# A third set of head tiles, with the low halves and the exponential's scale and bias moved to VectorE

## The chip, the cores and the metric

The kernel runs on one core of one Trainium2 chip. The metric is the device time of one execution in microseconds (us). The kernel before takes 824.26 us, the median of three runs (823.79 to 824.98).

## What is computed

Attention with a bucket mask over 2 x 8 heads of 768 positions and 64 dimensions, then two layers on its result (1536 tokens x 512):

```python
q_bits = (q @ proj > 0); k_bits = (k @ proj > 0)          # 6 bits each, a bucket number per position
scores = where(q_bucket == k_bucket, q @ k.T / 8, -1e9)
attn   = softmax(scores); x = attn @ v
h = x @ w_in;  g = (a0 + a1 h + a2 h^2 + a3 h^3) / (1 + |b0||h| + |b1| h^2);  x = g @ w_out
h = x @ w_in2; g = h * clip(h + 3, 0, 6) / 6;                                 out = g @ w_out2
```

Everything is fp32. The products of scores and of the layers are taken as sums of products of halves: a number is split into a rounded upper half (`hi`, type fp32r) and the rest (`lo`).

## The kernel before, in words

Five engines run programs of their own: TensorE (PE), VectorE (DVE), ScalarE (ACT), GpSimd (POOL) and SyncE (SP), which issues every DMA. Each program is written out in its order, and counting semaphores tie them together. There is no planner.

**Heads and tiles.** A head has six tiles of 128 query rows (`TILES`). Two heads are a pair, so there are eight pairs (0 to 7) and 96 tiles (n). Within a pair the tiles are j = 0 to 11, and j = 6 is the first tile of the second head; t is the tile within its head. The loop of every engine is `for i in pairs: for j in 12: step(i, j)`.

**One tile.** PE makes the scores of 128 x 768 into one of two score buffers `s_ps` (lines 775 to 779), once the exponential of tile n-2 has freed it. DVE takes the negated maximum (L595). POOL makes from it the scale (L378) and the bias (L381) of the exponential. ACT takes the exponential with its row sum (L432). DVE inverts the sum (L601), POOL multiplies by it (L387). Three tiles later (`TURN_LAG`) PE transposes the result (L786), and ACT and DVE each copy one half of it out of PSUM (L443, L611). In pair i PE also multiplies the transposed probabilities of pair i-1 by v (`weigh`, L803), in three pieces per head at t = 1, 3 and 5.

**Preparing a head.** The scores need four operand tiles per head: `q_main`, `k_main` (upper halves, with twelve more rows of signed mask bits) and `q_cross`, `k_cross` (which pair upper with lower halves). Before, there are two sets of them, one for each head of a pair. `raw` holds q in its partitions 0 to 63 and k in 64 to 127. ACT makes the upper half (`split_hi`, L426) at t = 0 of the head before, POOL the lower half (`split_lo`, L369) at t = 1. A DMA has to carry the parts to other partitions: SP's `place_head` (L261) issues three moves, waits until they have landed, and issues a fourth; `place_bits` (L275) issues four moves of mask bits. The bits come from `project` on PE (L763, at j = 7 for the next pair) and `threshold` on DVE (L590, at j = 8). The first scores of a head wait for all five DMAs of `main_in`.

**SP's order.** SP waits in order, so what stands behind a wait is late with it. Its loop over the heads h is: `place_head(h+1)`, v of the pair, an early load of weights, `place_bits(h+1)`, the next `raw`.

**Early weights.** The upper and lower halves of the first layer's weights are made in slots; before, five slots (`EARLY_SLOTS`) are made during pairs 2 to 6, one per pair: SP loads `w_raw` at the head of the pair, ACT takes the upper half at j = 4 and j = 8 (L459, `EARLY_AT`), and waits there until the load has landed. POOL makes the lower half (L394). The other slots are made in the first layer's first chunk.

**Layers.** After pair 7, PE runs 96 steps, each with `hidden` (L823 to L825) and `outputs` (L876).

Of the kernel before, what the change touches and what calls it, by code (L numbers as in the profile page):

```python
# [27 lines left out]
P = 128  # L28
# [5 lines left out]
def bucket_attention_and_two_mlps(nc, q, k, v, proj, w_in0, w_out0, poly_a, poly_b, w_in1, w_out1, out):  # L34
# [55 lines left out]
    with ctx:  # L90
# [29 lines left out]
        FREE_SLOTS = 5  # L120
# [5 lines left out]
        with attn:  # L126
            raw = [[sb(f"raw{e}{u}", [P, SEQ], F32, attn) for u in range(2)] for e in range(2)]
            pt_first = [[None, None], [None, None]]
            for g in range(2):
# [3 lines left out]
                for u in range(2)])  # L133
# [28 lines left out]
        bit_col_in = sem("bit_col_in")  # L162
        sel_made = sem("sel_made")
# [5 lines left out]
        v_in = [sem(f"v_in{e}") for e in range(2)]  # L169
        hi_made = sem("hi_made")  # L170
# [3 lines left out]
        moved_in = [sem(f"moved_in{u}") for u in range(2)]  # L174
        main_in = [sem(f"main_in{u}") for u in range(2)]
# [51 lines left out]

        def early_half(i, j):
# [16 lines left out]
        def _(sp):  # L245
# [14 lines left out]

            def place_head(h):  # L261

                u = h % 2
                sp.wait_ge(hi_made, h + 1)
                move(k_main[u][0:D, :], q_main[u][D:P, :]).then_inc(moved_in[u], 16)
                move(k_cross[u][0:D, :], q_main[u][D:P, :]).then_inc(moved_in[u], 16)
                if h > 0:
                    sp.wait_ge(lo_made, h + 1)
                    move(k_cross[u][D:P, :], q_cross[u][D:P, :]).then_inc(moved_in[u], 16)
                    sp.wait_ge(moved_in[u], 48 * (h // 2 + 1) - (16 if u == 0 else 0))  # L270
                move(q_cross[u][D:P, :], q_main[u][0:D, :]).then_inc(main_in[u], 16)
                if h == 0:
                    sp.wait_ge(moved_in[u], 32)

            def place_bits(h):  # L275

                i, u = divmod(h, 2)
                sp.wait_ge(bits_made, i + 2 if h else 1)
                for half in range(2):
                    cols = slice(HALF * half, HALF * (half + 1))  # L280
                    at = QUAD * (2 * u + half)
                    move(q_main[u][D:KROWS, cols], bits[at:at + MASKROWS, :]).then_inc(main_in[u], 16)
                    move(k_main[u][D:KROWS, cols], bits[at + MASKROWS:at + 2 * MASKROWS, :]).then_inc(main_in[u], 16)
# [11 lines left out]
            load_raw(0, 0)  # L295
            sp.dma_start(proj_raw[0:D, :], proj).then_inc(proj_in, 16)
            sp.dma_start(proj_raw[D:P, :], proj).then_inc(proj_in, 16)
            load_raw(0, 1)
            sp.wait_ge(sel_made, 4)
            for c in range(2):  # L300
                sp.dma_start(bit_col[:, c:c + 1], bit_row[0:1, c, :]).then_inc(bit_col_in, 16)
            place_head(0)
            load_v(0)
            place_bits(0)
            load_raw(1, 0)
            load_raw(1, 1)
            sp.dma_start(a_col[:, :], poly_a.partition_broadcast(P)).then_inc(poly_in, 16)
            sp.dma_start(b_raw[:, :], poly_b.partition_broadcast(P)).then_inc(poly_in, 16)

            for h in range(NHEAD):  # L310
                i, u = divmod(h, 2)
                if h + 1 < NHEAD:
                    place_head(h + 1)
                if u == 0 and i >= 1:
# [5 lines left out]
                if h >= 1 and h + 3 < NHEAD:  # L320
                    sp.wait_ge(lo_made, h)
                    sp.wait_ge(bits_dot, (h - 1) // 2 + 2)
                    load_raw((h + 3) // 2, (h + 3) % 2)
# [20 lines left out]
        def _(pool):  # L344
# [20 lines left out]
            def split_lo(h):  # L365

                u = h % 2
                alone(hi_made, h + 1)
                nc.gpsimd.tensor_tensor(q_cross[u][:, :], raw[h // 2 % 2][u][:, :], q_main[u][:, :].bitcast(F32),  # L369
                                        ALU.subtract).then_inc(lo_made, 1)  # L370

            def bias(n, j):


                r = j % 4
                neg = neg_max[:, r:r + 1]
                alone(maxed, n + 1)
                nc.gpsimd.tensor_scalar(exp_scale[:, r:r + 1], neg, MATCHED, SCALE, ALU.is_lt, ALU.mult)\  # L378
                    .then_inc(matched, 1)
                alone(matched, n + 1)  # L380
                nc.gpsimd.tensor_scalar(exp_bias[:, r:r + 1], neg, exp_scale[:, r:r + 1], 1.0, ALU.mult, ALU.mult)\  # L381
                    .then_inc(biased, 1)

# [13 lines left out]
            pool.wait_ge(lo_made, 1)  # L397
            for i in range(PAIRS):
                for j in range(2 * TILES):
                    h, n = 2 * i + j // TILES, 2 * TILES * i + j  # L400
                    bias(n, j)
                    if n >= 1:
                        normalise(n - 1, j - 1)
                    if j % TILES == 1 and h + 1 < NHEAD:
                        split_lo(h + 1)
# [11 lines left out]
        def _(act):  # L417

            nc.scalar.preload_act_table_set("natural_log_exp_and_others")
# [41 lines left out]
            def step(i, j):  # L461
# [8 lines left out]
                if t == 0 and h + 1 < NHEAD:  # L470
                    split_hi(h + 1)
# [459 lines left out]
```

## Time and profile before

| | us |
|---|---|
| Median of 3 runs | 824.26 (823.79 to 824.98) |
| The profiled execution | 824.72 |
| Its span, first to last instruction | 822.5 |
| PE busy | 769.8 (94%) |
| DVE busy | 465.1 (57%) |
| ACT busy | 439.0 (53%) |
| POOL busy | 240.4 (29%) |
| First scores | 15.28 |
| First `hidden` | 280.64 |

The busy time of PE counts matmuls with modelled ends and is no measure of its idle time; for that one reads where a matmul starts and what released it. The first 281 us are attention, where the engines work by turns; the rest is dense on PE.

### The profile page before, as it was taken

To read this page: it belongs to the slowest core of one execution; us is meant where nothing else is said; L and a number is where in the kernel's file an instruction comes from. 1 tells how busy PE (TensorE), PEld (TensorE's weight loads), DVE (VectorE), ACT (ScalarE), POOL (GpSimd) and SP (SyncE) were. 2 spreads that over 40 slices of the span, in tenths; PEclk is the share of its full clock that TensorE was granted. 3 is DMA by queue.
4 is the path that set the end of the run, shared out by engine and by line. 5 is a ranking of instruction groups with operands and counts; after the bars stand their busy time and mean duration, and the time that the engine had idled before them with its cause. 6 is when DMAs were issued, how large, how long until landed. Compare 5 with 4: busy or idle time off the path is not lost.

```text
span 822.5 us, 11290 instructions
## 1 busy us (share of the span) xinstructions
PE 769.8 (94%) x3712; PEld 595.7 (72%) x3712; DVE 465.1 (57%) x777; ACT 439.0 (53%) x781; POOL 240.4 (29%) x379
## 2 busy tenths in 40 slices
PE   3889898798979799999999999999999999999998
PEld 1665565465655558888888888888888888888886
DVE  3656565465645458888988898984222322232223
ACT  1656665576656648877766688984221222212221
POOL 1756676576756414420000024443000000000000
PEclk9989999989989999999999999999999999999999
DMA  5233434434333002320000013331000100000001
GB/s 147 53 91 84 126 75 116 112 87 115 93 98 88 1 26 84 96 77 0 1 0 0 0 31 99 101 103 52 1 0 1 51 0 0 0 34 18 1 1 51
DMA packets 35451, 43.50 MB, mean 53 GB/s; under 512 B 4496, under 2 KB 23696, under 8 KB 35408
## 3 DMA queue, kind: packets, MB, share of 16 engines
q1 hardware_dynamic: 35408, 42.95, 19.1%
q8 instruction: 24, 0.39, 0.2%
q14 instruction: 19, 0.16, 0.1%
HBM read 26.22 MB, written 3.15 MB: 36 GB/s over the span
## 4 chain that ended last, share of the span: by engine, by line
PE 78%; DMA 7%; SPq 5%; POOL 4%; DVE 3%; issue 2%; ACT 1%; POOLq 0%; ACTq 0%; DVEq 0%
PE y_ps L876 32%; PE h_ps L823 11%; PE h_ps L824 11%; PE h_ps L825 11%; PE o_ps L803 4%; PE t_ps L786 4%; DMA k_cross<-q_cross 3%; PE s_ps L776 3%; SPq L259 3%; PE s_ps L777 2%; DMA k_main<-bits 2%; POOL q_cross L369 2%; DVE neg_max L595 2%; POOL probs L387 1%; SPq L255 1%
## 5 line engine op out<-in xcount | busy, mean ns | idle before, releaser
L823 PE MATMUL h_ps<-x_hi,slot 128*128 (+1 forms) x384 | 149.7, 390 | 1.5 <-DVE x_lo L617 1.5
L824 PE MATMUL h_ps<-x_lo,slot 128*128 (+1 forms) x384 | 149.4, 389 | 0.0
L825 PE MATMUL h_ps<-x_hi,slot 128*128 (+1 forms) x384 | 149.4, 389 | 0.0
L394 POOL TENSOR_TENSOR slot<-w_raw,slot 128x512 fp32r<-128x512 f32 x64 | 81.7, 1294 | 215.6 <-ACT slot L459 215.5
L672 DVE SCALAR_TENSOR_TENSOR t_abs<-t_abs,h_ps 128x512 f32<-128x512 f32 x48 | 33.0, 688 | 187.2 <-ACT t_abs L496 187.2
L496 ACT ACTIVATE t_abs<-h_ps,three_col 128x512 f32<-128x512 f32 x48 | 33.1, 690 | 192.1 <-PE h_ps L825 192.1
L595 DVE TENSOR_REDUCE neg_max<-s_ps 128x1 f32<-128x768 f32 x96 | 91.7, 955 | 76.7 <-PE s_ps L777 76.5
L432 ACT ACTIVATE probs<-s_ps,exp_bias,exp_scale 128x768 f32<-128x768 f32 x96 | 95.2, 991 | 62.0 <-POOL exp_bias L381 61.1
L876 PE MATMUL y_ps<-g_hi,slot 128*128 128x512 f32 x384 | 126.1, 389 | 0.0
L876 PE MATMUL y_ps<-slot,g_hi 128*128 128x512 f32 x384 | 118.2, 389 | 0.0
L776 PE MATMUL s_ps<-k_cross,q_cross 128*128 128x512 f32 x192 | 80.0, 417 | 36.2 <-DMA k_main<-bits 24.3
L786 PE MATMUL t_ps<-ident,probs 128*128 128x128 f32 x576 | 90.9, 291 | 6.0 <-ACT pt_second L443 3.2
L387 POOL TENSOR_SCALAR probs<-probs,row_inv 128x768 f32<-128x768 f32 x96 | 87.5, 911 | 20.1 <-DVE row_inv L601 19.7
L776 PEld LDWEIGHTS s_ps<-k_cross,q_cross 128*128 128x128 f32 x192 | 39.9, 208 | 72.7 <-DMA k_main<-bits 33.3
L823 PEld LDWEIGHTS h_ps<-x_hi,slot 128*128 128x128 f32 x384 | 72.1, 188 | 17.3 <-DVE x_lo L617 1.8
L876 PEld LDWEIGHTS y_ps<-g_hi,slot 128*128 128x128 f32 x384 | 72.1, 188 | 15.4 <-DVE g_lo L678 0.2
L825 PEld LDWEIGHTS h_ps<-x_hi,slot 128*128 128x128 f32 x384 | 72.0, 188 | 15.1
L876 PEld LDWEIGHTS y_ps<-slot,g_hi 128*128 128x128 f32 x384 | 72.0, 188 | 14.9
L824 PEld LDWEIGHTS h_ps<-x_lo,slot 128*128 128x128 f32 x384 | 72.1, 188 | 14.7
L786 PEld LDWEIGHTS t_ps<-ident,probs 128*128 128x128 f32 x576 | 70.9, 150 | 13.3 <-issue 12.5
L876 PE MATMUL y_ps<-g_lo,slot 128*128 128x512 f32 x192 | 74.7, 389 | 0.0
L876 PE MATMUL y_ps<-slot,g_lo 128*128 128x512 f32 x192 | 74.7, 389 | 0.0
(68 smaller groups left out, 1189.0 us busy)
## 6 DMA issues: line engine op xcount, KB each, us to landing
w_raw<-in_moe_w_in SPq DMA_DIRECT2D x32, 256.0 KB, 2.7
w_raw<-in_moe_w_out SPq DMA_DIRECT2D x32, 256.0 KB, 2.8
raw<-in_q SPq DMA_DIRECT2D x16, 192.0 KB, 3.1
raw<-in_k SPq DMA_DIRECT2D x16, 192.0 KB, 3.3
k_main<-q_main SPq DMA_DIRECT2D x16, 192.0 KB, 2.5
k_cross<-q_main SPq DMA_DIRECT2D x16, 192.0 KB, 2.9
q_cross<-q_main SPq DMA_DIRECT2D x16, 192.0 KB
v_nat<-in_v SPq DMA_DIRECT2D x16, 192.0 KB, 2.7
```

Of the source, the lines that this page charges most:

```text
L387: nc.gpsimd.tensor_scalar(probs[j % 4][:, :], probs[j % 4][:, :], row_inv[:, r:r + 1], 1.0, ALU.mult, ALU.mult).then_inc(normed, 1)
L394: nc.gpsimd.tensor_tensor(slots[f][:, j, 1, :], w_raw[j][:, :], slots[f][:, j, 0, :].bitcast(F32), ALU.subtract).then_inc(w_lo_made, 1)
L432: nc.scalar.activation(probs[j % 4][:, :], s_ps[j % 2][:, 0:SEQ], ACT.Exp, scale=exp_scale[:, r:r + 1], bias=exp_bias[:, r:r + 1], accum_o ...
L496: nc.scalar.activation(t_abs[b][:, :], h_ps[b][:, :], ACT.Relu, bias=three_col[:, :])\
L595: nc.vector.tensor_reduce(neg_max[:, j % 4:j % 4 + 1], s_ps[j % 2][:, 0:SEQ], AX.X, ALU.max, negate=True)\
L672: nc.vector.scalar_tensor_tensor(t_abs[b][:, :], t_abs[b][:, :], 6.0, h_ps[b][:, :], ALU.min, ALU.mult).then_inc(g_made, 1)
L776: mm(s_ps[j % 2][:, c0:c1], q_cross[u][:, rows], k_cross[u][:, c0:c1], start=True, stop=False)
L786: last = nc.tensor.transpose(t_ps[half][:, P * s:P * (s + 1)], probs[n % 4][:, c:c + P], ident[:, :])
L823: mm(h_ps[b][:, :], w_hi, x_hi[:, kt, cols], start=(kt == 0), stop=False)
L824: mm(h_ps[b][:, :], w_hi, x_lo[:, kt, cols], start=False, stop=False)
L825: last = mm(h_ps[b][:, :], w_lo, x_hi[:, kt, cols], start=False, stop=(kt == KT - 1))
L876: last = mm(y_ps[d][:, :], still, moving, start=(f == 0 and a == 0), stop=(f == FT - 1 and a == 2))
```

## The change

- There are three sets of head tiles (`SETS = 3`), taken in turn by the head's number. Every step of the preparation moves one head earlier: during head h, head h+2 is made ready. `project` moves from j = 7 to j = 1 and `threshold` from j = 8 to j = 2.
- `split_lo` and `bias` (the scale and bias) move from POOL to DVE. The bias stands right behind the maximum.
- SP's loop over h becomes: v, the whole of `place_head(h+2)` with its bits (two moves of k bits ahead of the wait for the landing, two moves of q bits behind it), `raw` of h+6, and then the early weights.
- One slot of weights less fits: `EARLY_SLOTS` 4, made in pairs 3 to 6.
- The first head is made without moves between partitions: q and k are also loaded swapped into `raw[1][0]`, and ACT and DVE copy from there. ACT issues some of the first DMAs. `raw` of heads 2 and 3 is loaded behind `place_head(1)`.
- At the end the transposes of tile 93 go ahead of the first `hidden`, and the copies of turned tiles go earlier on ACT and DVE; the last x but two is made at j = 10 in place of 11.

```diff
-    PROJECT_AT = TILES + 1
+    PROJECT_AT = 1
+    SETS = 3
-    LAST_X = {5: 2 * PAIRS - 4, 11: 2 * PAIRS - 3}
-    EARLY_SLOTS = 5
+    LAST_X = {5: 2 * PAIRS - 4, 10: 2 * PAIRS - 3}
+    EARLY_SLOTS = 4
...
+            def place_keys(h):
+                c = h % SETS
                 sp.wait_ge(hi_made, h + 1)
+                move(k_main[c][0:D, :], q_main[c][D:P, :]).then_inc(moved_in[c], 16)
+                move(k_cross[c][0:D, :], q_main[c][D:P, :]).then_inc(moved_in[c], 16)
+            def place_head(h):
+                c = h % SETS
+                place_keys(h)
+                sp.wait_ge(bits_made, h // 2 + 2)
+                place_bits(sp, h, 1)
+                sp.wait_ge(lo_made, h + 1)
+                move(k_cross[c][D:P, :], q_cross[c][D:P, :]).then_inc(moved_in[c], 16)
+                sp.wait_ge(moved_in[c], moved(h))
+                move(q_cross[c][D:P, :], q_main[c][0:D, :]).then_inc(main_in[c], 16)
+                place_bits(sp, h, 0)
...
+            place_bits(sp, 0, 0)
             load_v(0)
-            place_bits(0)
+            place_head(1)
+            sp.wait_ge(first_k, 2)
             load_raw(1, 0)
             load_raw(1, 1)
+            load_raw(2, 0)
+            load_raw(2, 1)
...
             for h in range(NHEAD):
                 i, u = divmod(h, 2)
-                if h + 1 < NHEAD:
-                    place_head(h + 1)
                 if u == 0 and i >= 1:
                     load_v(i)
+                if h + 2 < NHEAD:
+                    place_head(h + 2)
+                if h + 6 < NHEAD:
+                    load_raw((h + 6) // 2, h % 2)
                 if u == 0 and EARLY_PAIR <= i < EARLY_PAIR + EARLY_SLOTS:
                     load_weights(0, i - EARLY_PAIR)
-                if h + 1 < NHEAD:
-                    place_bits(h + 1)
...
 (ACT)
-                if t == 0 and h + 1 < NHEAD:
-                    split_hi(h + 1)
+                if t == 0 and h + 2 < NHEAD:
+                    split_hi(h + 2)
...
+            act.wait_ge(swapped_in, 32)
+            for to in (k_main, k_cross):
+                nc.scalar.activation(to[0][0:D, :], raw[1][0][0:D, :], ACT.Copy).then_inc(first_k, 1)
...
             act.wait_ge(hi_made, 1)
+            split_hi(1)
...
 (DVE)
                 maximum(n, j)
+                bias(n, j)
                 if n >= 1:
                     invert(n - 1, j - 1)
...
                 if j == PROJECT_AT + 1 and i + 1 < PAIRS:
                     threshold(i + 1)
+                if t == 1 and h + 2 < NHEAD:
+                    split_lo(h + 2)
...
 (PE, behind the last step)
+            for half in range(2):
+                turn_probs(NTILE - 3, half)
             hidden(0, 0, 0, 0)
-            for n in (NTILE - 3, NTILE - 2):
-                for half in range(2):
-                    turn_probs(n, half)
+            for half in range(2):
+                turn_probs(NTILE - 2, half)
```

**SP, pair 3 (its v load to the `raw` load of the second head's turn).** Before:

```order
67 L255 DMA v_nat<-in_v 128x384 [waits pv_done]
68 L255 DMA v_nat<-in_v 128x384
69 L293 DMA w_raw<-in_moe_w_in 128x4x128
70 L293 DMA w_raw<-in_moe_w_out 128x512
71 L259 DMA q_main<-bits 12x384 [waits bits_made]
72 L259 DMA k_main<-bits 12x384
```

With the change, the same place (v of pair 3, then head 8's moves):

```order
83 L267 DMA v_nat<-in_v 128x384 [waits pv_done]
84 L267 DMA v_nat<-in_v 128x384
85 L271 DMA k_main<-q_main 64x768 [waits hi_made]
86 L271 DMA k_cross<-q_main 64x768
87 L287 DMA k_main<-bits 12x384 [waits bits_made]
88 L287 DMA k_main<-bits 12x384
89 L271 DMA k_cross<-q_cross 64x768 [waits lo_made]
90 L271 DMA q_cross<-q_main 64x768 [waits moved_in2]
91 L287 DMA q_main<-bits 12x384 x2
92 L260 DMA raw<-in_q 64x768
93 L261 DMA raw<-in_k 64x768
94 L309 DMA w_raw<-in_moe_w_in 128x4x128
```

The weights stood right behind v; now they stand behind nine or ten more issues and behind four waits, of which `bits_made` is the threshold at j = 2 of the same pair.

**ACT, the first rows with the change, up to the first exponential (L429).**

```order
7 L477 ACTIVATE k_main<-raw 64x768 [waits swapped_in]
8 L477 ACTIVATE k_cross<-raw 64x768
9 L481 DMA k_main<-bits 12x384 [waits bits_made]
10 L481 DMA k_main<-bits 12x384
11 L423 ACTIVATE q_main<-raw 128x768 [waits raw_in01,hi_made]
12 L423 ACTIVATE q_main<-raw 128x768 [waits raw_in10]
13 L429 ACTIVATE probs,row_sum<-s_ps,exp_bias,exp_scale 128x768 [waits biased] x3
```

Before, the first exponential stood right behind row 11's counterpart; now a second split, of head 2, which waits for `raw[1][0]`, stands ahead of it.

**DVE, one tile with the change (t = 1 of the second head, with `split_lo` behind it).**

```order
44 L599 TENSOR_REDUCE neg_max<-s_ps 128x1 [waits scored]
45 L608 TENSOR_SCALAR exp_scale<-neg_max 128x1 [waits maxed]
46 L611 TENSOR_SCALAR exp_bias<-neg_max,exp_scale 128x1 [waits matched]
47 L616 RECIPROCAL row_inv<-row_sum 128x1 [waits exped]
48 L626 COPY pt_first<-t_ps 128x3x128 [waits turned]
49 L594 TENSOR_TENSOR q_cross<-raw,q_main 128x768 [waits hi_made]
```

Before, a tile on DVE was the first, fourth and fifth of these rows; the second, third and (once per head) the last are new there.

## Rows read from the trace of the kernel before

**Rows 1.** What PE waited for, 0 to 330 us: total us, times, longest.

```profile
PE s_ps L776 <- DMA k_main<-bits: 24.3, 8, 6.7
```

**Rows 2.** PE's timeline: start us, us, line, tile [idle before <-releaser].

```profile
46.09 0.80 PE L776 MATMUL s_ps<-k_cross,q_cross 128*128 128x512 f32 x1 [3.52 <-DMA k_main<-bits]
...
53.46 0.50 PE L776 MATMUL s_ps<-k_cross,q_cross 128*128 128x512 f32 x1
...
96.29 0.47 PE L776 MATMUL s_ps<-k_cross,q_cross 128*128 128x512 f32 x1 [3.37 <-DMA k_main<-bits]
...
102.23 0.85 PE L763 MATMUL p_ps<-raw,proj_pair 128*32 128x384 f32 x8
103.01 0.50 PE L776 MATMUL s_ps<-k_cross,q_cross 128*128 128x512 f32 x1
...
112.09 0.50 PE L776 MATMUL s_ps<-k_cross,q_cross 128*128 128x512 f32 x1
...
117.14 0.50 PE L776 MATMUL s_ps<-k_cross,q_cross 128*128 128x512 f32 x1
...
129.27 0.47 PE L776 MATMUL s_ps<-k_cross,q_cross 128*128 128x512 f32 x1 [2.98 <-ACT probs L432]
...
136.27 0.50 PE L776 MATMUL s_ps<-k_cross,q_cross 128*128 128x512 f32 x1
...
247.86 0.50 PE L776 MATMUL s_ps<-k_cross,q_cross 128*128 128x512 f32 x1
```

**Rows 3.** The window view: us, then busy us of PE to POOL, granted clock, DMA.

```profile
46.00:52.00 6.00, 5.91 (x22) 5.01 (x24) 2.99 (x6) 2.06 (x4) 1.68 (x5) 0.50 0.45 123
```

**Rows 4.** Timeline of SP and ACT in pair 3 (SPq: an issue).

```profile
123.61 0.44 SPq L293 DMA_DIRECT2D w_raw<-in_moe_w_in  x1
...
124.65 0.81 SPq L259 DMA_DIRECT2D q_main<-bits  x1
...
127.53 0.63 ACT L459 ACTIVATE slot<-w_raw 128x512 fp32r<-128x512 f32 x1 [4.00 <-DMA w_raw<-in_moe_w_in]
...
128.46 0.60 SPq L249 DMA_DIRECT2D raw<-in_k  x1
```

**Rows 5.** DMA issues, 118 to 152 us: KB each, median us from issue to landing.

```profile
k_cross<-q_cross SPq DMA_DIRECT2D x2, 192.0 KB, 2.5
...
raw<-in_k SPq DMA_DIRECT2D x2, 192.0 KB, 3.3
...
w_raw<-in_moe_w_in SPq DMA_DIRECT2D x1, 256.0 KB, 3.9
```

**Rows 6.** The page's DMA issues: the same load over the whole span.

```profile
w_raw<-in_moe_w_in SPq DMA_DIRECT2D x32, 256.0 KB, 2.7
```

**Rows 7.** DVE's timeline: two rows of one tile, and the threshold behind project.

```profile
79.75 0.96 DVE L595 TENSOR_REDUCE neg_max<-s_ps 128x1 f32<-128x768 f32 x1 [0.91 <-PE s_ps L777]
80.62 0.15 DVE L601 RECIPROCAL row_inv<-row_sum 128x1 f32<-128x1 f32 x1
...
81.15 0.55 DVE L611 COPY pt_second<-t_ps 128x384 f32<-128x384 f32 x1
...
105.43 0.67 DVE L590 TENSOR_SCALAR bits<-p_ps,bit_col 128x384 fp32r<-128x384 f32 x1
```

**Rows 8.** The timeline of the first 24 us.

```profile
16.94 0.96 DVE L595 TENSOR_REDUCE neg_max<-s_ps 128x1 f32<-128x768 f32 x1 [7.44 <-PE s_ps L777]
...
18.83 0.99 ACT L432 ACTIVATE probs<-s_ps,exp_bias,exp_scale 128x768 f32<-128x768 f32 x1 [10.81 <-POOL exp_bias L381]
```

**Rows 9.** The end of attention: PE's timeline, and of the chain that ended last its L803.

```profile
263.84 0.50 PE L776 MATMUL s_ps<-k_cross,q_cross 128*128 128x512 f32 x1 [1.75 <-DMA k_main<-bits]
...
278.14 0.97 PE L786 MATMUL t_ps<-ident,probs 128*128 128x128 f32 x6
...
294.35 0.88 PE L786 MATMUL t_ps<-ident,probs 128*128 128x128 f32 x6
...
297.99 4.02 PE p_ps L803 x24
```

More of the change, by code:

```diff
@@ L132, in bucket_attention_and_two_mlps @@
                 [sb(f"{name}{u}", [P, SEQ], F32R, attn) for name in ("q_cross", "k_cross", "q_main", "k_main")]
-                for u in range(2)])
+                for u in range(SETS)])
             bits = sb("bits", [P, HALF], F32R, attn)
@@ L173, in bucket_attention_and_two_mlps @@
         bits_made = sem("bits_made")
-        moved_in = [sem(f"moved_in{u}") for u in range(2)]
-        main_in = [sem(f"main_in{u}") for u in range(2)]
+        first_k = sem("first_k")
+        moved_in = [sem(f"moved_in{s}") for s in range(SETS)]
+        main_in = [sem(f"main_in{s}") for s in range(SETS)]
         scored = sem("scored")
@@ L259, in move, with place_bits @@
                 return sp.dma_start(dst.bitcast(F32), src.bitcast(F32))
[L261 to L263 removed]
+            def place_keys(h):
+                c = h % SETS
                 sp.wait_ge(hi_made, h + 1)
[L265 to L278, printed above, removed]
+                move(k_main[c][0:D, :], q_main[c][D:P, :]).then_inc(moved_in[c], 16)
+                move(k_cross[c][0:D, :], q_main[c][D:P, :]).then_inc(moved_in[c], 16)
+            def place_bits(queue, h, side):
+                c, at = h % SETS, 2 * QUAD * (h % 2) + MASKROWS * side
+                to = (q_main, k_main)[side][c]
                 for half in range(2):
                     cols = slice(HALF * half, HALF * (half + 1))
[L281 to L283 removed]
+                    rows = slice(at + QUAD * half, at + QUAD * half + MASKROWS)
+                    queue.dma_start(to[D:KROWS, cols].bitcast(F32), bits[rows, :].bitcast(F32)).then_inc(main_in[c], 16)
+            def place_head(h):
[8 more added lines that the diff above has]
+                place_bits(sp, h, 0)
             def load_weights(m, f):
@@ L363, in _ @@
                                     base=0, pattern=[[-1, P]], channel_multiplier=1).then_inc(sel_made, 1)
[L365 to L382, printed above, removed]
             def normalise(n, j):
@@ L417, in _ @@
         def _(act):
+            act.dma_start(raw[0][0][D:P, :], k_dram[dram_head(0, 0), :, :]).then_inc(raw_in[0][0], 16)
+            act.dma_start(proj_raw[0:D, :], proj).then_inc(proj_in, 16)
+            act.dma_start(raw[1][0][0:D, :], k_dram[dram_head(0, 0), :, :]).then_inc(swapped_in, 16)
+            act.wait_ge(sel_made, 4)
+            for c in range(2):
+                act.dma_start(bit_col[:, c:c + 1], bit_row[0:1, c, :]).then_inc(bit_col_in, 16)
             nc.scalar.preload_act_table_set("natural_log_exp_and_others")
@@ L424, in split_hi @@
                 act.wait_ge(raw_in[i % 2][u], 32 * (i // 2 + 1))
-                after(act, scored, TILES * (h - 1))
-                nc.scalar.activation(q_main[u][:, :], raw[i % 2][u][:, :], ACT.Copy).then_inc(hi_made, 1)
+                after(act, scored, TILES * (h - SETS + 1))
+                nc.scalar.activation(q_main[h % SETS][:, :], raw[i % 2][u][:, :], ACT.Copy).then_inc(hi_made, 1)
             def exponentials(n, j):
@@ L476, in step @@
                     split_weights(0, f, (half,))
+            act.wait_ge(swapped_in, 32)
+            for to in (k_main, k_cross):
+                nc.scalar.activation(to[0][0:D, :], raw[1][0][0:D, :], ACT.Copy).then_inc(first_k, 1)
+            act.wait_ge(bits_made, 1)
+            for half in range(2):
+                cols, rows = slice(HALF * half, HALF * (half + 1)), QUAD * half + MASKROWS
+                act.dma_start(k_main[0][D:KROWS, cols].bitcast(F32), bits[rows:rows + MASKROWS, :].bitcast(F32))                    .then_inc(main_in[0], 16)
             act.wait_ge(hi_made, 1)
+            split_hi(1)
             for i in range(PAIRS):
@@ L775, in scores @@
                 for c0, c1 in ((0, BANK), (BANK, SEQ)):
-                    mm(s_ps[j % 2][:, c0:c1], q_cross[u][:, rows], k_cross[u][:, c0:c1], start=True, stop=False)
-                    last = mm(s_ps[j % 2][:, c0:c1], q_main[u][0:KROWS, rows], k_main[u][0:KROWS, c0:c1],
+                    mm(s_ps[j % 2][:, c0:c1], q_cross[c][:, rows], k_cross[c][:, c0:c1], start=True, stop=False)
+                    last = mm(s_ps[j % 2][:, c0:c1], q_main[c][0:KROWS, rows], k_main[c][0:KROWS, c0:c1],
                               start=False, stop=True)
@@ L849, in _ @@
             pe.wait_ge(x_ready, 2 * PAIRS - 2)
+            for half in range(2):
+                turn_probs(NTILE - 3, half)
             hidden(0, 0, 0, 0)
-            for n in (NTILE - 3, NTILE - 2):
-                for half in range(2):
-                    turn_probs(n, half)
+            for half in range(2):
+                turn_probs(NTILE - 2, half)
             weigh(PAIRS - 1, 0, tuple(range(TILES)))
```

75 lines of the change are left out of this document (47 added, 28 removed).

## The prediction

> **What bounds the kernel now.** I read the waits of PE first, then PE's timeline at the heads' first tiles, then the engines behind each wait. Behind attention PE runs without a gap and the change leaves its work alone, so every gain or loss lies in attention. There PE's largest wait is for `k_main<-bits`, the last DMA of a head's placing: 24.3 us in 8 waits [rows 1]. The pattern is: the second head of pair 2 starts at 96.29 after 3.37 us of idleness, while from 103.01 to 112.09 four tiles take 9.08, or 4.54 per two tiles, with no wait at all [rows 2]. So without waits PE's own work is the bound: 6 x 4.54, plus 0.78 for project (102.23 to 103.01), plus 0.5 at a pair's first two tiles (112.09 to 117.14 is 5.05), **28.5 us for a pair**. Pairs 1 and 2 together take 66.0 (46.09 to 112.09), pairs 3 to 6 together 135.8 (112.09 to 247.86) [rows 2].
>
> A second wait hides behind the first. In pair 3 the second head starts at 129.27, released not by a DMA but by ACT's exponential [rows 2]. ACT had stood 4.00 us at j = 4 for the early weights, which SP issued at 123.61, 11.5 us behind the pair's first scores; they landed at 127.53, and 1.74 us later (half a split, then the exponential of tile 4) PE went on [rows 2, 4]. Such a wait costs more than its length: the two tiles from 129.27 to 136.27 take 7.00, less 0.78 for project 6.2, against 4.54. After the wait at 46.09 the granted clock stood at 0.50, the lower level of 1.2 GHz, from the first tile [rows 3], and two tiles took 7.4 (to 53.46).
>
> **The change part by part.** Times below are from PE's first scores of the pair, S.
>
> *Third set of tiles.* Per pair SP has about 20 us of issues and landings (two heads at 8.7, v, weights), under 28.5, and begins a head early, so a head's placing is ready with over 10 us to spare. The waits for bits go. Pairs 1 and 2, which have no early weights now, become 2 x 28.5 = 57.0: **-9.0**.
>
> *Early weights.* They now stand behind all of `place_head(h+2)` and `raw`. The gate is the threshold at j = 2. Project begins at S+5.05 on PE's pace; from project to the end of the threshold are 3.20 + 0.67 (102.23 to 105.43) [rows 2, 7], and 0.34 for two small operations now ahead of it: S+9.3. Then SP issues two k bits (0.81 each, with gaps 1.66) [rows 4], and a move that lands 2.5 after its issue [rows 5]: S+13.4. Then 0.5 for the last move, 1.66 for two q bits, and 1.2 for `raw` in pairs 3 and 4 (0.60 each) [rows 4]; `raw` of h+6 ends with head 15, so pairs 5 and 6 have none. The weights are issued at S+16.8 and S+15.6, against 11.5 now. They land 3.9 later in pair 3's row [rows 5], 2.7 in the median over the span, mostly without other traffic [rows 6]; I take 3.9 behind `raw` and 3.3 without: S+20.7 and S+18.9. With the 1.74 of ACT, tile 6 starts at S+22.4 and S+20.6, some 7 and 5 us after PE has run out of work. For the restart the bounds are 6.2 and 7.4 [rows 2]. I take 7.4, because that row's clock was already down when PE resumed, as it should be after a longer wait. The last four tiles take 9.1, as from 103.01 to 112.09. So pairs 3 and 4 take 38.9 and pairs 5 and 6 37.1, together 152.0 against 135.8: **+16.2**. What is saved at heads is more than given back here.
>
> *Bias and low halves on DVE.* Today the exponential starts 1.89 behind the maximum's start (16.94 to 18.83) [rows 8]. On DVE two small operations of 0.15, each behind a wait on its own engine of some 0.03, make it about 1.4. In steady pairs this is worth nothing, because PE's own work ends last. DVE's load per tile, start to start, is 0.87 for the maximum, 0.07 for the reciprocal and 0.46 for the copy of 0.55 [rows 7], 1.4 in all, and becomes 1.8; a head adds 0.95 for the low half, a pass over 768 columns as the maximum is [rows 8], and 0.8 for the rest, or 12.6 against PE's 14.2. It is hidden, with 1.6 to spare. If that cover goes, each us too much per head costs up to 14 us.
>
> The Trainium skill, "VectorE: DVE Perf Modes", section "The DRAIN you can't avoid", says that the next operation does not start until the pipe is empty, and that a semaphore between two adds nothing. By full spans a tile costs 2.0 and a head 13.6, still under PE's, and pair 0, where DVE ends last, would be 2 us longer: the sum would be 821. The trace speaks against the first half: the reciprocal starts at 80.62, while the maximum lasts to 80.71 [rows 7].
>
> *Start.* q, k and the bits go in without moves, and the first scores could start near 10.4. But ACT must split head 2 before the first exponential, and that waits for `raw[1][0]`. SP issues it only behind `place_head(1)`. On the same durations: threshold at 7.4; two bits to 9.1, v to 10.0, two moves to 11.2, two bits to 12.8, a landing at 15.3, a move and two bits to 17.5, k issued at 18.1, landed 3.3 later [rows 5] at 21.4. The split takes 0.85, so the first exponential starts at 22.25, not 18.83 [rows 8]: 3.4 later. From it to pair 1's first scores are 27.3 today, 4.3 of them waits for bits (0.82 at the second head, 3.52 at 46.09) [rows 2]. The shorter way to the exponential gives 0.5 on each of six rounds of two tiles, DVE's two low halves take 1.7 back. 22.25 + 27.3 - 4.3 - 1.3 = 43.9, against 46.09: **-2.2**. Bounds: 42 and 46.
>
> *Pair 7 and the end.* Its second head waits 1.75 [rows 9] and restarts at the lower clock (1.7 by 6.2 less 4.54): **-3.4**. Today the transposes end at 278.8, and then PE waits for x, and twice for turned tiles behind ACT's and DVE's reading of `hidden`, until tile 95 is transposed at 294.35. With the new order the same work is: 0.4 for the normalised tile 93, 3.64 for six transposes and a `hidden` (294.35 to 297.99), 0.7 for six more, 4.02 for 24 matmuls of `weigh` [rows 9], or 287.5: **-6.9**. Below nothing it can't come; half of it is the other bound. One slot less is ready at the first layer; the others follow one per step of 5.44 us and lie some 6 us ahead of their use, so it costs nothing. If the first were later by more than that, PE would wait for each.
>
> Sum: -2.2 - 9.0 + 16.2 - 3.4 - 6.9 = -5.3. The profiled execution took 824.72 (span 822.5), 0.5 above the median; 824.26 - 5.3 gives **819.0**.
>
> **Rivals.**
> - *Still later weights: slower.* At ACT's wait at j = 4 of pairs 3 to 6. Each us by which the weights land later costs 4 us; from 1.3 us on, S+22, the kernel is slower than before. A threshold held up by DVE's larger load (up to 1) and 1 us more to land than in the row make 2 us: 827. For it speaks that four waits stand ahead; against it, that DVE has slack then.
> - *The wait for weights is hidden.* If PE had other work, pairs 3 to 6 would take 28.5 each, and the time would be 819 - 38 = 781. Against it stands 129.27, released by the exponential right behind the split [rows 2].
> - *DVE starts nothing before the operation ahead has ended.* Then a tile costs 2.0 there, and pair 0 is 2 us longer: 821. Against it: 80.62 lies before 80.71 [rows 7].
> - *No difference.* Half of the end's gain and the start's fail to come (+4.5): 823.5.
> - *The change doesn't do what it says.* Heads still wait for bits, since SP is one queue. Against it: 20 us of work in 28.5. Such waits would lie inside the weights' wait in pairs 3 to 6, so only pairs 1 and 2 lose their 9.0: 828.
>
> **How the numbers follow.** A difference within 0.2% (822.6 to 825.9) can't be told from none. The forecast has 0.60: its own range is 810 (restarts at 6.2, -4.8, and weights 1 us earlier, -4) to 824 (start and end at their other bounds). DVE held back has 0.05, at 821; that is the skill's DRAIN rule. Later weights have 0.17, no difference 0.11, heads that still wait 0.03, the hidden wait 0.04. The range, 808 to 828, leaves out the hidden wait and the far ends. Of the forecast 0.03 lies in "same". Faster 0.57 + 0.05 + 0.04 = 0.66, same 0.14, slower 0.20.
>
> **What would show it.** In the new profile: no wait for bits from tile 6 on; four waits of ACT for `w_raw` of 7 to 9 us, and behind each a wait of PE for the exponential of 5 to 8 us; weights issued 15 to 17 us behind the pair's first scores; the first scores near 10.4 but the first exponential at 22; pairs 1 and 2 at 28.5 each, DVE near 12.6 busy us per head. The prediction is wrong if the four waits are short, if pairs 1 and 2 take over 30 us (then DVE bounds), or if the first layer waits for slots.

## The result and the profile after

The changed kernel takes **834.8 us**, the median of four runs (833.84 to 835.36), against 824.62 for the kernel before, measured beside it (four runs, 823.79 to 828.26). The ratio is 1.0118, with a 95% interval of 1.0100 to 1.0135: slower by 1.2%, or 10.2 us between the medians. The prediction, 819.0 in a range of 808 to 828, had the wrong sign. The profiled execution took 835.36 us.

The page of the changed kernel: the span, the busy times, and in 40 slices the granted clock of PE.

```profile
span 833.6 us, 11076 instructions
...
PE 769.8 (92%) x3712; PEld 591.5 (71%) x3712; DVE 514.5 (62%) x985; ACT 439.1 (53%) x783; POOL 170.6 (20%) x172
...
PEclk9999998979899999999999999999999999999999
```

PE is busy for the same 769.8 us as before, in a span that is 11.1 us longer; POOL has lost 70 us of work and DVE has gained 49. So what counts is where PE stood. PE's timeline of the changed kernel, in the columns of [rows 2]: the first scores of pairs 1, 2 and 3, the second head of pair 3, its third tile, pair 4, pair 7, the first `hidden` and the first `outputs`.

```profile
47.90 0.47 PE L810 MATMUL s_ps<-k_cross,q_cross 128*128 128x512 f32 x1
...
79.28 0.51 PE L810 MATMUL s_ps<-k_cross,q_cross 128*128 128x512 f32 x1
...
110.98 0.50 PE L810 MATMUL s_ps<-k_cross,q_cross 128*128 128x512 f32 x1
...
133.58 0.77 PE L810 MATMUL s_ps<-k_cross,q_cross 128*128 128x512 f32 x1 [6.38 <-ACT probs L429]
...
140.02 0.51 PE L810 MATMUL s_ps<-k_cross,q_cross 128*128 128x512 f32 x1
...
150.02 0.50 PE L810 MATMUL s_ps<-k_cross,q_cross 128*128 128x512 f32 x1
...
265.34 0.50 PE L810 MATMUL s_ps<-k_cross,q_cross 128*128 128x512 f32 x1
...
297.83 0.48 PE L857 MATMUL h_ps<-x_hi,slot 128*128 128x512 f32 x1
...
315.91 0.39 PE L911 MATMUL y_ps<-g_hi,slot 128*128 128x512 f32 x1
```

In the trace of the kernel before, the first `outputs` row is this one:

```profile
304.83 0.39 PE L876 MATMUL y_ps<-g_hi,slot 128*128 128x512 f32 x1
```

Read with [rows 2], these rows divide the 11.1 us between the two traces among four stretches, and leave nothing for the fifth:

| stretch | before | after | difference | predicted |
|---|---|---|---|---|
| start, to pair 1's first scores | 46.09 | 47.90 | +1.8 | -2.2 |
| pairs 1 and 2 | 66.00 | 63.08 | -2.9 | -9.0 |
| pairs 3 to 6 | 135.77 | 154.36 | +18.6 | +16.2 |
| pair 7, to the first `outputs` | 56.97 | 50.57 | -6.4 | -10.3 |
| from there to the end | 517.7 | 517.7 | 0.0 | 0.0 |

Two waits stand behind this table. PE's and ACT's waits of the changed kernel from 0 to 330 us, in the columns of [rows 1]:

```profile
ACT slot L456 <- DMA w_raw<-in_moe_w_in: 27.8, 4, 8.2
PE s_ps L810 <- ACT probs L429: 23.1, 5, 6.7
...
PE t_ps L820 <- DVE pt_first L626: 8.4, 18, 1.5
PE t_ps L820 <- DVE pt_second L626: 7.8, 20, 0.8
...
PE s_ps L810 <- DMA k_main<-bits: 4.1, 1, 4.1
```

The waits for bits are down from 8 to 1, the very first. In their place stand four waits of ACT for `w_raw`, of about 7 us each, with PE behind it at the exponential: that was forecast. The 38 waits of PE's transposes for DVE's copies, 16.2 us in all, were not.

The first of the two in pair 3. SP's issues and ACT's half of the weights, from the timeline of the changed kernel:

```profile
120.74 1.59 SPq L287 DMA_DIRECT2D k_main<-bits  x2
...
128.33 0.59 SPq L309 DMA_DIRECT2D w_raw<-in_moe_w_in  x1
...
131.84 0.63 ACT L456 ACTIVATE slot<-w_raw 128x512 fp32r<-128x512 f32 x1 [7.84 <-DMA w_raw<-in_moe_w_in]
```

From the pair's first scores (110.98) the k bits go out at 9.8, the weights at 17.4, ACT gets them at 20.9, and tile 6 starts at 22.6. The prediction had 9.3, 16.8, 20.7 and 22.4.

The second, in a steady pair. DVE, ACT and PE in one tile of pair 2 of the changed kernel, in order of time:

```profile
86.52 0.96 DVE L599 TENSOR_REDUCE neg_max<-s_ps 128x1 f32<-128x768 f32 x1 [1.14 <-PE s_ps L811]
...
87.51 0.15 DVE L608 TENSOR_SCALAR exp_scale<-neg_max 128x1 f32<-128x1 f32 x1
...
87.69 0.49 PE L820 MATMUL t_ps<-ident,probs 128*128 128x128 f32 x3
87.70 0.21 DVE L611 TENSOR_SCALAR exp_bias<-neg_max,exp_scale 128x1 f32<-128x1 f32 x1
87.83 0.15 DVE L616 RECIPROCAL row_inv<-row_sum 128x1 f32<-128x1 f32 x1
87.90 0.54 DVE L626 COPY pt_second<-t_ps 128x384 f32<-128x384 f32 x1
87.94 1.00 ACT L429 ACTIVATE probs<-s_ps,exp_bias,exp_scale 128x768 f32<-128x768 f32 x1 [0.61 <-DVE exp_bias L611]
...
88.58 0.52 PE L820 MATMUL t_ps<-ident,probs 128*128 128x128 f32 x3 [0.40 <-DVE pt_second L626]
```

DVE is idle for 1.14 us ahead of the maximum, and yet PE waits for DVE. The copy that frees the transposes' buffer stands behind the maximum and three small operations, so it starts 1.38 us behind the maximum's start, and PE's next three transposes wait 0.40 us for it. DVE has time enough; it is its order that PE meets.

### The profile page after: what moved, and what is told of

Its sections match the earlier page's. It is cut to its first block, busy times and chain, and to the rows that moved or that the text cites. A ratio compares the mean times of both kernels' runs of the same rounds, so it can differ in the third digit from the quotient of the medians.

```text
span 833.6 us, 11076 instructions
## 1 busy us (share of the span) xinstructions
PE 769.8 (92%) x3712; PEld 591.5 (71%) x3712; DVE 514.5 (62%) x985; ACT 439.1 (53%) x783; POOL 170.6 (20%) x172
## 4 chain that ended last, share of the span: by engine, by line
PE 79%; DVE 11%; DMA 4%; SPq 3%; issue 2%; ACT 1%; ACTq 0%; DVEq 0%
PE y_ps L911 31%; PE h_ps L857 10%; PE h_ps L858 10%; PE h_ps L859 10%; PE o_ps L837 6%; DVE neg_max L599 5%; PE t_ps L820 3%; PE s_ps L810 3%; PE s_ps L811 2%; SPq L287 2%; DMA k_cross<-q_cross 2%; DMA w_raw<-in_moe_w_in 1%; DVE pt_first L626 1%; DVE pt_second L626 1%; DVE exp_scale L608 1%
## 5 line engine op out<-in xcount | busy, mean ns | idle before, releaser
L599 DVE TENSOR_REDUCE neg_max<-s_ps 128x1 f32<-128x768 f32 x96 | 91.4, 952 | 42.8 <-PE s_ps L811 42.8
L429 ACT ACTIVATE probs<-s_ps,exp_bias,exp_scale 128x768 f32<-128x768 f32 x96 | 95.2, 991 | 39.5 <-DVE exp_bias L611 38.8
L810 PE MATMUL s_ps<-k_cross,q_cross 128*128 128x512 f32 x192 | 78.8, 410 | 27.5 <-ACT probs L429 23.1
L820 PEld LDWEIGHTS t_ps<-ident,probs 128*128 128x128 f32 x576 | 68.7, 147 | 30.0 <-issue 29.9
```

The source lines that it names most:

```text
L429: nc.scalar.activation(probs[j % 4][:, :], s_ps[j % 2][:, 0:SEQ], ACT.Exp, scale=exp_scale[:, r:r + 1], bias=exp_bias[:, r:r + 1], accum_o ...
L599: nc.vector.tensor_reduce(neg_max[:, j % 4:j % 4 + 1], s_ps[j % 2][:, 0:SEQ], AX.X, ALU.max, negate=True)\
L810: mm(s_ps[j % 2][:, c0:c1], q_cross[c][:, rows], k_cross[c][:, c0:c1], start=True, stop=False)
L820: last = nc.tensor.transpose(t_ps[half][:, P * s:P * (s + 1)], probs[n % 4][:, c:c + P], ident[:, :])
```

## The experiments

The theory after this reading: the four waits for weights come from SP's order alone, and the copy waits from DVE's order alone, not from DVE's load. The rivals: weights would be late in any order; the low halves fill DVE; the bias on DVE is too much work wherever it stands. All experiments are edits of the changed kernel, four to ten runs each, beside runs of the kernel before, whose medians in these batches lay between 824.2 and 825.4.

**Weights first (SP).**

```diff
                 if u == 0 and i >= 1:
                     load_v(i)
+                if u == 0 and EARLY_PAIR <= i < EARLY_PAIR + EARLY_SLOTS:
+                    load_weights(0, i - EARLY_PAIR)
                 if h + 2 < NHEAD:
                     place_head(h + 2)
                 if h + 6 < NHEAD:
                     load_raw((h + 6) // 2, h % 2)
-                if u == 0 and EARLY_PAIR <= i < EARLY_PAIR + EARLY_SLOTS:
-                    load_weights(0, i - EARLY_PAIR)
```

> The changed kernel with one edit: SP loads the early weights right behind v, ahead of place_head(h+2). Theory A (the weights' wait is what pairs 3 to 6 lose, 37.6 to 40.1 us each where pairs 1 and 2 take 31.4 and 31.7): ACT's waits for w_raw vanish, pairs 3 to 6 take 31.7 each, time 834.8 - 27.6 = 807. Rival (the second half of those pairs would wait for something else, the bits of the next heads, which are now issued 1 us later, or for the same exponential): 820 or more, with another wait of PE at tile 6.

Measured: 807.82 us, 0.9798 of before (0.9781 to 0.9815). PE's waits with weights first, 0 to 330 us:

```profile
PE t_ps L820 <- DVE pt_first L626: 9.8, 22, 1.5
PE t_ps L820 <- DVE pt_second L626: 8.3, 21, 0.8
...
PE s_ps L810 <- ACT probs L429: 0.4, 1, 0.4
```

PE's wait for the exponential is gone, 23.1 to 0.4, and the head's placing is not late for it: there is no new wait for bits. Pairs 3 to 6 take 126.8 us in this trace (112.33 to 239.10) instead of 154.4. Two lines moved are worth 27.0 us between the medians. The copy waits are all still there.

**The same from ACT's side.** SP's order stays, and ACT takes the weights at j = 8 and 10.

```diff
-    EARLY_AT = (4, 8)
+    EARLY_AT = (8, 10)
```

> The changed kernel with EARLY_AT (8, 10) in place of (4, 8): SP loads the weights where it did, ACT takes them four and two tiles later. They land at S+20.9, tile 8's turn comes near S+21. If only the lateness against ACT's turn costs, the waits nearly vanish as with the weights first (807.8): 808 to 812. If the load itself disturbs (traffic beside the head's moves), it stays above 815.

Measured: 807.81 us, 0.9807 (0.9769 to 0.9844), the same as with weights first to 0.01 us in the median. ACT's waits for `w_raw<-in_moe_w_in` are gone from its list. So the late load itself cost nothing. What cost was that ACT stood in line for it, with the exponentials behind it. Where one of the two is mended, there is nothing left for the other.

**Copy first (DVE).** The scale and bias stay on DVE, but behind the copy, and so does the reciprocal.

```diff
                 maximum(n, j)
+                if n >= TURN_LAG:
+                    take_turned(n - TURN_LAG)
                 bias(n, j)
...
-                if n >= TURN_LAG:
-                    take_turned(n - TURN_LAG)
```

> The changed kernel with one edit: on DVE the copy of the turned tile stands right behind the maximum, ahead of scale and bias. Theory A (the order on DVE: PE waits 0.4 us for the copy at every second tile, because two small operations stand ahead of it): two tiles take 4.54 again in place of 4.97, PE's waits for pt_first and pt_second of DVE go, pairs 1, 2 and 7 gain 2.6 each and the second halves of pairs 3 to 6 0.9 each, about 12 in all: 823. Rival (DVE has too much work, whatever its order): no change, 834 to 835.

Measured: 820.38 us, 0.9953 (0.9938 to 0.9968), 14.4 under the changed kernel. DVE's timeline with the copy first, one tile of pair 2:

```profile
88.64 0.96 DVE L599 TENSOR_REDUCE neg_max<-s_ps 128x1 f32<-128x768 f32 x1 [0.39 <-PE s_ps L811]
89.51 0.55 DVE L626 COPY pt_first<-t_ps 128x384 f32<-128x384 f32 x1
```

The copy starts 0.87 behind the maximum, not 1.38. Pairs 1 and 2 take 29.0 us each in this trace (48.30, 77.32, 106.36), against 31.5 with the bias first and 28.5 in the prediction, and no wait of PE's transposes for DVE is left in the list. DVE still does all the work that the change gave it. One thing beside the order differs: the low half takes 0.94 us on DVE here and mostly 1.54 in the changed kernel (see the last section). The run with the low halves on POOL, below, shows that this is not what mends the pairs.

**Bias back on POOL.** `bias` moves from DVE's loop into POOL's, ahead of `normalise`; on POOL it is `tensor_scalar` with a second multiplier of 1.0. The calls, without the functions that move with them:

```diff
 (POOL)
+                    bias(n, j)
...
 (DVE)
                 maximum(n, j)
-                bias(n, j)
```

> The changed kernel with scale and bias back on POOL, and nothing else. If their place on DVE costs the 0.4 us at every second tile, PE's waits for DVE's copy go and the time is 823 to 825 (the exponential starts 0.5 later, which is hidden). If the bias on DVE is worth something that I don't see, it is over 835.

Measured: 822.65 us, 0.9971 (0.9960 to 0.9983). Pairs 1 and 2 take 28.9 and 29.0 us. It mends the pairs as copy first does.

**Low halves back on POOL, the bias still on DVE.**

```diff
 (POOL)
+                    if j % TILES == 1 and 2 * i + j // TILES + 2 < NHEAD:
+                        split_lo(2 * i + j // TILES + 2)
...
 (DVE)
-                if t == 1 and h + 2 < NHEAD:
-                    split_lo(h + 2)
```

> The changed kernel with the low halves (split_lo of heads 2 to 15) back on POOL, bias left on DVE. Theory A (order of bias and copy): nearly nothing, 833 to 835, since only one tile per head has the low half behind it. Rival (DVE's load): 14 low halves of 0.9 us off DVE give up to 12 us: 823.

Measured: 833.64 us, 1.0103 (1.0080 to 1.0125), hardly under the changed kernel's 834.8. Pairs 1 and 2 take 31.3 and 31.5 us: taking the low halves from DVE (12 of them, 17.9 us, from 48 to 285 us in the changed kernel) mends next to nothing while the bias stands ahead of the copy. Less load on DVE in its old order leaves the pairs at 31.4, and the same operations in a new order bring them to 29.0: that rules out DVE's load as the cause.

**Both back on POOL.** What is left is the third set with SP's new order, the new start and the new end.

> The changed kernel with both moved pieces back on POOL: scale and bias, and the low halves of heads 2 to 15. What is left of the change is the third set with its order on SP, the start and the end. If the loss of 3 us per pair came from the bias's place alone, this equals the run with only the bias back (822.65): 821 to 824. If the low half on DVE is worth something of its own, it is slower than that by a few us.

Measured: 822.14 us, 0.9982 (0.9960 to 1.0004), no different from the kernel before as far as this tells. Pairs 1 and 2 take 28.8 and 29.0. So without its DVE part the change gives to the heads and the end what it takes elsewhere: in this trace pairs 1 and 2 are 8.1 us shorter than in the kernel before and pair 7 with the end 8.7, while pairs 3 to 6 are 10.0 longer and the start 3.0.

**The old end**: the order of transposes and copies as before, and `LAST_X` back at 11. ACT's and DVE's copies go back to their places too, which is left out here.

```diff
-    LAST_X = {5: 2 * PAIRS - 4, 10: 2 * PAIRS - 3}
+    LAST_X = {5: 2 * PAIRS - 4, 11: 2 * PAIRS - 3}
...
 (PE)
-            for half in range(2):
-                turn_probs(NTILE - 3, half)
             hidden(0, 0, 0, 0)
-            for half in range(2):
-                turn_probs(NTILE - 2, half)
+            for n in (NTILE - 3, NTILE - 2):
+                for half in range(2):
+                    turn_probs(n, half)
```

> The changed kernel with the old order at the end (transposes and copies of tile 93 behind the first hidden, the last x but two at j = 11). From the traces the new order gave 6.1 us between the first hidden and the first outputs (24.35 against 18.24) and about as much as nothing before it: 841. If the order is worth nothing and the difference came from something else: 835.

Measured: 841.89 us, 1.0220 (1.0180 to 1.0261). The end's new order is worth 7.1 us, against the 6.9 of the prediction. (The expectation's 24.35 and 18.24 are 24.19 and 18.08 in the traces, with the same difference.) PE's waits with the old end, from 294 to 325 us:

```profile
PE t_ps L820 <- DVE pt_second L626: 2.1, 2, 1.7
PE t_ps L820 <- ACT pt_second L440: 1.8, 1, 1.8
PE h_ps L857 <- DVE x_lo L632: 1.2, 1, 1.2
```

Of these 5.1 us all but 0.4 are the waits that the prediction named: for x (1.2), and twice for turned tiles behind the reading of `hidden` (1.7 and 1.8). In the changed kernel there are 1.8 us of waits behind 283 us.

**The start: `raw` of heads 2 and 3 ahead of `place_head(1)`.** The second split of ACT stands ahead of the first exponential and waits for it.

```diff
             load_v(0)
-            place_head(1)
             sp.wait_ge(first_k, 2)
+            sp.wait_ge(hi_made, 1)
             load_raw(1, 0)
             load_raw(1, 1)
+            place_head(1)
```

> The changed kernel with the loads of raw[1][0] and raw[1][1] issued ahead of place_head(1). Theory (ACT's split of head 2, ahead of the first exponential, waits for that load): the first exponential starts near 18 in place of 25.06, and all behind it comes 7 us earlier: 828. Rival (place_head(1), now 2.5 us later, makes head 1 late by more): PE waits for bits at tile 6 and half of it is lost, 831.

Measured: 831.21 us, 1.0083 (1.0057 to 1.0110), 3.6 under the changed kernel. First the rows of the changed kernel at its start: the first bits, SP's k of `raw[1][0]`, the second split and the first exponential.

```profile
9.27 1.67 SPq L287 DMA_DIRECT2D q_main<-bits  x2
...
20.84 0.60 SPq L261 DMA_DIRECT2D raw<-in_k  x1
...
24.31 0.84 ACT L423 ACTIVATE q_main<-raw 128x768 fp32r<-128x768 f32 x1 [11.72 <-DMA raw<-in_k]
...
25.06 0.98 ACT L429 ACTIVATE probs<-s_ps,exp_bias,exp_scale 128x768 f32<-128x768 f32 x1
```

And the timeline with `raw` first (its line numbers are one higher, by the added wait):

```profile
17.23 0.97 ACT L430 ACTIVATE probs<-s_ps,exp_bias,exp_scale 128x768 f32<-128x768 f32 x1
...
21.68 1.59 SPq L287 DMA_DIRECT2D q_main<-bits  x2
...
24.62 0.68 DVE L588 TENSOR_SCALAR bits<-p_ps,bit_col 128x384 fp32r<-128x384 f32 x1 [2.22 <-DMA q_main<-bits]
...
27.27 0.87 PE L821 MATMUL t_ps<-ident,probs 128*128 128x128 f32 x3 [2.47 <-DVE pt_first L627]
```

The first exponential comes 7.8 us earlier, at 17.23, but pair 1 only 3.6 earlier, at 44.31. The rest turned into another wait: `place_head(1)` is later by its place on SP, its q bits land late, DVE's threshold waits 2.22 us until the tile of bits is free, and the copy behind it on DVE makes PE wait 2.47. The expectation's 828 was too low for want of that chain; how much of the difference each of its links takes was not tried. The 831 is the number of the expectation's rival, but the wait that the rival named is not there: PE has no wait for bits behind the first.

**Together.** Weights first and copy first:

> The changed kernel with two edits: the weights right behind v on SP, and the copy ahead of the bias on DVE. If the two causes are independent and each pair then runs at PE's own pace (29.0 us as pairs 1 and 2 in the run with the copy first), pairs 1 to 7 and 0 gain what they did apart, and pairs 3 to 6 2.7 each once more over the weights alone: 807.8 - 2.7 * 7 - 1 = 788.

Measured: 789.57 us, 0.9571 (0.9552 to 0.9589). Alone the two gave 27.0 and 14.4 us, together 45.2. The traces show where most of the 3.8 more come from. With weights first the pairs from 1 to 6 take 31.7 us (the first of them 31.9), and with both 29.0, so the copy's order is worth 2.7 in each; with late weights it gave 7.6 in pairs 3 to 6 together (154.4 to 146.8), 1.9 in each, or 3.0 less. The likely reason is that part of a pair's copy waits lay inside PE's wait for the exponential; no run tried that alone. PE's waits with both edits, from 30 to 330 us:

```profile
PE s_ps L810 <- ACT probs L429: 2.9, 6, 0.8
PE t_ps L820 <- ACT pt_second L440: 2.5, 7, 1.1
PE t_ps L820 <- ACT pt_first L440: 1.6, 7, 0.2
```

**Is the bias on DVE worth anything then?** Weights first, with scale and bias on POOL:

> The changed kernel with the weights first on SP (as in e1) and scale and bias back on POOL (as in e3). It tells what making the bias on VectorE is worth once the queue's order is right, against e6 (789.57), where the bias stays on VectorE behind the copy. Theory (the bias only has to be out of the copy's way, and VectorE has a little more room without it): e2 and e3 stood at 820.4 and 822.65, POOL's bias 2.3 behind, so e7 about 792, in 789.5 to 795. Rival (a bias on POOL comes late enough to hold up the exponentials, and once the weights no longer cover it, that shows on every tile): over 797. Other rival (the bias on VectorE buys nothing, and its four small operations there cost): under 788.5.

Measured: 792.69 us, 0.9619 (0.9586 to 0.9652): 3.1 behind the bias on DVE behind the copy. In the traces 2.7 of it are there at the first `hidden` (252.50 against 255.17), and 2.1 by pair 2 (77.75 against 79.83); from there pairs 2 to 6 take 29.0 in both, and pair 7 gives the last 0.7. The shorter way to the exponential pays in pairs 0, 1 and 7, and nothing in a steady pair. In pairs 0 and 1 PE waits for the exponential for 2.9 us with the bias on DVE and 4.8 with it on POOL; what makes the difference in pair 7 was not looked into.

**With `raw` first too:**

> The same two edits and the loads of raw[1] ahead of place_head(1). Expected: the kernel with the two edits less what the loads gave alone, about 7: 781.

Measured: 784.71 us, 0.9512 (0.9492 to 0.9532). The best of the study, 40.3 us under the kernel before as measured beside it (825.02) and 50.1 under the change. Pair 1 starts at 43.27 (48.74 without), and six pairs take 29.0 each. The gain over the two edits is 4.9, where 7 had been expected.

**And the projection's matrix loaded first,** on both queues, since PE's first project had waited for it. SP's part; ACT's is alike:

```diff
+            sp.dma_start(proj_raw[D:P, :], proj).then_inc(proj_in, 16)
             sp.dma_start(raw[0][0][0:D, :], q_dram[dram_head(0, 0), :, :]).then_inc(raw_in[0][0], 16)
             sp.dma_start(raw[1][0][D:P, :], q_dram[dram_head(0, 0), :, :]).then_inc(swapped_in, 16)
-            sp.dma_start(proj_raw[D:P, :], proj).then_inc(proj_in, 16)
```

> The same three edits, and proj ahead of raw on both queues at the start. In the changed kernel proj landed at 6.39, 1.4 later than before, behind five loads of 192 KB; first in its queues it should land near 3.5, project then waits for raw alone (about 5), and everything comes 1.5 to 2 us earlier than with the three edits. If raw then lands later by as much, nothing is gained.

Measured: 785.50 us, 0.9522 (0.9503 to 0.9541): a miss, no gain. Of its timeline, DVE's copy of the matrix and the first move of bits:

```profile
2.96 0.51 DVE L580 TENSOR_SCALAR proj_pair<-proj_raw 64x6 f32<-64x6 f32 x4 [2.06 <-DMA proj_raw<-in_proj]
...
9.83 1.68 SPq L287 DMA_DIRECT2D q_main<-bits  x2
```

The matrix is there 3.2 us earlier (2.96, and 6.15 without the edit), and now q and k are late: PE's project waits for them until 5.51 and again for 1.9 us. The q bits go out at 9.83, and at 9.03 without the edit.

## Why the prediction was wrong

**Third set of tiles: right.** No wait for bits is left but the first, and a head's placing stays out of the way even with the weights ahead of it on SP. The rival that heads still wait for bits falls.

**Early weights: right in mechanism, +18.6 for +16.2.** Weights issued, landed and tile 6 started within 0.6 us of the working, and the second heads of pairs 3 to 6 start at 22.6, 23.0, 20.6 and 20.7 us (22.4 and 20.6 predicted). The restart at the lower clock took 6.4 in pair 3 (133.58 to 140.02), within the bounds of 6.2 and 7.4 and below the 7.4 taken, and about 7.1 in the others. What was missed are the last four tiles: 10.0 (140.02 to 150.02) in place of 9.1, four times, which is the copy wait again; the shorter restarts took back about half of it. The rival of still later weights, at 827, gave the right sign for the wrong reason.

**Pairs 1 and 2: the step that failed, -2.9 for -9.0.** The 57.0 us came from PE's own pace, and the cover for DVE's new work was a head's sum of "12.6 against PE's 14.2. It is hidden, with 1.6 to spare". That is a sum of loads, and as such it was near: DVE is busy for 26.4 and 25.4 us in pairs 1 and 2, about 13 per head. PE doesn't wait for DVE's load but for one instruction in its program, the copy, and the change had put some 0.5 us of other instructions ahead of it. Copy first takes the same DVE operations to 58.1 us for the two pairs, which is 5.0 of the 6.1 missed. The other 1.1 is a second, smaller miss: without waits a pair takes 29.0 and not 28.5, since the first two tiles of its second head take 5.05 as well (63.32 to 68.37 with copy first), where the sum had 4.54. The sentence "In steady pairs this is worth nothing, because PE's own work ends last" asked only whether the exponential gains by an earlier bias, and not who stands behind the bias. This one term runs through the whole: 2.7 us in each of pairs 1 to 6 with weights first, and 3.0 in pair 7 (222.99 to 270.57 with both edits, 47.6 us; 50.6 in the changed kernel).

One of the prediction's own signs of being wrong came true here, "if pairs 1 and 2 take over 30 us (then DVE bounds)": they took 31.4 and 31.7. DVE does bound them, but by its order and not by its load.

A third slip in the same sum: the low half was taken at 0.95 and is mostly 1.54 (below). Its whole stay on DVE costs 1.2 us of the median, so this did not decide.

**Start: +1.8 for -2.2.** The chain was the right one: the exponential waits for the second split, and that for SP's turn. Its first link was off. The threshold was put at 7.4, and the q bits go out at 9.27 (and the first scores come at 13.96, not near 10.4); then k is issued at 20.84 (18.1) and the exponential starts at 25.06 (22.25). From it to pair 1 are 22.8 us, where 21.7 had been worked out.

**Pair 7 and the end: -6.4 for -10.3.** The end's order is worth 7.1 by the old-end run, as worked out. Of the -3.4 for pair 7 only 0.3 came (32.78 us to the first `hidden` before, 32.49 after), because the copy waits are there too: 3.4 us in the list of PE's waits from 265 to 316 us, 3.0 by the run with both edits.

**DVE starting nothing before the operation ahead has ended: not so here.** The reciprocal starts at 87.83 and the bias ahead of it lasts to 87.91. But `exp_scale` starts 0.03 behind the maximum's end, and `exp_bias` 0.04 behind `exp_scale`'s; each of them waits for the result of the one ahead. The prediction took from the Trainium skill ("VectorE: DVE Perf Modes", "The DRAIN you can't avoid") that the next operation waits for an empty pipe, and that a semaphore adds nothing. The same section adds that a next operation that is not held starts earlier, and the trace agrees with that: the reciprocal starts 0.08 before the bias ends. On the semaphore it differs: the two operations behind a wait start 0.11 to 0.12 later, against the end of the one ahead, than the reciprocal does.

The four terms miss by 4.0, 6.1, 2.4 and 3.9, together the 16.4 us between -5.3 and +11.1.

## What to carry to other kernels

Before calling added work on an engine hidden, find the instruction on that engine which the bounding engine waits for, and count what the change puts ahead of it: half a microsecond ahead of a copy cost 2.7 us per pair on an engine that stood idle for 42.8 us ahead of its maxima (45 of the 96 tiles), and the same work behind it cost a steady pair nothing. A queue's order can do the same: four waits of ACT for late loads, 27.8 us together, cost the kernel 27.0, and either issuing the loads earlier or taking them later removed all of it. Experiments on a change with several parts should also be run together, since one wait hides part of another (27.0 and 14.4 us alone, 45.2 together).

## What the runs showed of the hardware

**DVE and POOL exclude each other over the low half.** The operation reads two SBUF tiles (`raw` and `q_main`). Its minimum, median and maximum duration in ns in the changed kernel:

```profile
L594 DVE TENSOR_TENSOR q_cross<-raw,q_main x15: 939/1540/1545, 12.6 to 254.4; 128x768 fp32r<-128x768 f32 x15
```

With copy first:

```profile
L594 DVE TENSOR_TENSOR q_cross<-raw,q_main x15: 937/939/959, 12.7 to 243.6; 128x768 fp32r<-128x768 f32 x15
```

Two places in the changed kernel's timeline, POOL's multiply beside it:

```profile
84.43 0.95 DVE L594 TENSOR_TENSOR q_cross<-raw,q_main 128x768 fp32r<-128x768 f32 x1
...
84.61 1.55 POOL L382 TENSOR_SCALAR probs<-probs,row_inv 128x768 f32<-128x768 f32 x1 [1.73 <-DVE row_inv L616]
...
115.96 0.91 POOL L382 TENSOR_SCALAR probs<-probs,row_inv 128x768 f32<-128x768 f32 x1 [1.39 <-DVE row_inv L616]
...
116.13 1.54 DVE L594 TENSOR_TENSOR q_cross<-raw,q_main 128x768 fp32r<-128x768 f32 x1
```

Whichever starts first keeps its usual time (0.95 or 0.91), and the other takes about 0.6 more. In the changed kernel POOL starts first 12 times of 15. With copy first DVE's low half starts first whenever they meet, 0.28 to 0.31 ahead (once 0.63), and POOL's multiply takes 1.41 to 1.43 (once 1.09). The time added is each time some 0.13 less than what was left of the first. The Trainium skill says so too ("SBUF — State Buffer", "SBUF: two separate sides"): the pair of ports that VectorE and GpSimd share is an exclusive lock, which the first holds for its whole instruction, and a VectorE operation with two SBUF inputs takes it against a GpSimd operation that reads SBUF. The trace agrees, but for the 0.13. The maximum and the copy, which read PSUM, keep their 0.95 and 0.55 beside the same multiply.

**Restarting after a long wait of PE.** The window view of the changed kernel, behind the waits of pairs 3 and 4: us, then busy us of PE to POOL, granted clock, DMA.

```profile
133.50:135.50 2.00, 1.92 (x7) 1.75 (x8) 0.86 (x3) 2.00 (x5) 1.66 (x2) 0.50 0.00 0
173.00:175.00 2.00, 2.00 (x7) 1.81 (x8) 0.87 (x3) 2.00 (x5) 1.75 (x2) 0.50 0.00 0
```

After 6.4 and 6.8 us of idleness PE comes back at 0.50, the level of 1.2 GHz, and the first two tiles take 6.4 and 7.2 us, where the same two tiles take 5.4 in pair 1 (63.77 to 69.20). Over the four pairs that is about 6 us (27.7 against 21.7). With weights first the mean granted clock of the run is 0.998, against 0.982, so about 6 of its 27 us are this.
